# Attention heads ahead of two MLPs, Trainium2: the TensorE's fp32r products and its fp32 products in one stretch each per head, with four score chunks of 384, 384, 384 and 448 columns

## The reference

```
B, H, S, D = 4, 8, 576, 64
scores = where(causal, -1e9, (q @ k.T) / sqrt(D))
a = exp(scores - scores.max(-1));  a /= a.sum(-1) + 1e-9
local = a @ v
phi(x) = where(x > 0, x, exp(x) - 1) + 1
mem_out = (phi(q) @ M_prev) / (phi(q) @ z_prev + 1e-6)
g = sigmoid(beta)
attn = g * mem_out + (1 - g) * local          # [B, S, H * D]
x = (s * relu(attn @ w_in)**2 + b) @ w_out     # first MLP
out = layernorm(solu(x @ v_in)) @ v_out        # second MLP
```

## Time and profile before

| | us |
|---|---|
| median of 3 runs | 821.39 (821.21 to 822.12) |
| profiled execution, its own time | 821.17 |
| profiled execution, span | 819.4 |
| TensorE busy (matmuls) | 810.7 |
| VectorE busy | 510.4 |
| ScalarE busy | 339.6 |
| GpSimd busy | 339.1 |

### The profile page before, as it was taken

One profiled execution on the slowest core, in us unless ns is written; L12 is line 12 of the kernel. 1 busy time (PEld: TensorE's weight loads), 2 busy tenths in 40 slices (PEclk: granted clock), 3 DMA queues, 4 the chain that ended last, 5 costly groups with the idle time before them and its releaser, 6 DMA issues.

```text
span 819.4 us, 14574 instructions
## 1 busy us (share of the span) xinstructions
PE 810.7 (99%) x5630; PEld 704.2 (86%) x5630; DVE 510.4 (62%) x1052; ACT 339.6 (41%) x608; POOL 339.1 (41%) x453
## 2 busy tenths in 40 slices
PE   8999999999999999999999999999999999999998
PEld 7788888888888888888888899999998888888886
DVE  7877777776588653333433353346688977777762
ACT  6766776675422232222322232233436434333431
POOL 6667676676899930000000000005268844443300
PEclk9999999999999999999999999999999999999999
DMA  8587777866134320000000000000111000000001
GB/s 152 128 178 154 173 167 155 178 142 144 53 103 116 95 73 1 1 1 0 1 1 0 1 1 1 1 1 1 52 51 52 26 27 26 26 14 27 26 14 51
DMA packets 86371, 49.45 MB, mean 60 GB/s; under 512 B 65056, under 2 KB 73248, under 8 KB 86304
## 3 DMA queue, kind: packets, MB, share of 16 engines
q1 hardware_dynamic: 83760, 47.94, 24.3%
q10 hardware_dynamic: 2544, 0.59, 0.4%
HBM read 27.28 MB, written 4.72 MB: 39 GB/s over the span
## 4 chain that ended last, share of the span: by engine, by line
PE 96%; DVE 1%; issue 0%; ACT 0%; POOL 0%; POOLq 0%
PE ps_h L1297 8%; PE ps_y L1313 8%; PE ps_h L1298 8%; PE ps_h L1299 8%; PE ps_y L1314 8%; PE ps_y L1312 8%; PE ps_v L678 5%; PE ps_s L591 4%; PE ps_r L1766 4%; PE ps_r L1764 4%; PE ps_r L1765 4%; PE ps_hid L1701 4%; PE ps_hid L1699 4%; PE ps_hid L1700 3%; PE ps_x L657 3%; PE ps_x L658 3%
## 5 line engine op out<-in xcount | busy, mean ns | idle before, releaser
L1414 DVE TENSOR_TENSOR xT<-xT 128x512 f32<-128x512 f32 (+1 forms) x80 | 61.2, 765 | 127.7 <-ACT xT L1372 127.7
L1598 POOL TENSOR_TENSOR win<-stage,win 128x512 fp32r<-128x512 f32 x2 | 2.6, 1296 | 282.4 <-ACT win L1833 282.4
L1314 PE MATMUL ps_y<-g_hi,wout 128*128 128x512 f32 (+1 forms) x320 | 117.5, 367 | 0.0
L1313 PE MATMUL ps_y<-g_lo,wout 128*128 128x512 f32 (+1 forms) x320 | 117.5, 367 | 0.0
L1312 PE MATMUL ps_y<-g_hi,wout 128*128 128x512 f32 (+1 forms) x320 | 117.4, 367 | 0.0
L1378 ACT ACTIVATE g_hi<-xT 128x512 fp32r<-128x512 f32 (+1 forms) x80 | 47.3, 591 | 135.0 <-DVE xT L1416 135.0
L1297 PE MATMUL ps_h<-x_hi,win 128*128 128x512 f32 (+1 forms) x280 | 103.0, 368 | 0.0
L1299 PE MATMUL ps_h<-x_hi,win 128*128 128x512 f32 (+1 forms) x280 | 102.8, 367 | 0.0
L1298 PE MATMUL ps_h<-x_lo,win 128*128 128x512 f32 (+1 forms) x280 | 102.8, 367 | 0.0
L1372 ACT ACTIVATE xT<-ps_h 128x512 f32<-128x512 f32 (+1 forms) x80 | 44.3, 554 | 139.0 <-PE ps_h L1299 137.2
L1419 DVE TENSOR_TENSOR g_lo<-xT,g_hi 128x512 fp32r<-128x512 f32 (+1 forms) x80 | 65.1, 813 | 52.6 <-ACT g_hi L1378 52.6
(11 more groups left out here) (220 smaller groups left out, 1814.6 us busy)
## 6 DMA issues: line engine op xcount, KB each, us to landing
stacked<-cut SPq DMA_DIRECT2D x56, 288.0 KB, 4.8
out<-res SPq DMA_DIRECT2D x18, 256.0 KB, 2.0
v_raw<-in_v SPq DMA_DIRECT2D x32, 128.0 KB, 2.7
stage<-in_moe_w_in SPq DMA_DIRECT2D x16, 256.0 KB, 2.8
stage<-in_moe_w_out SPq DMA_DIRECT2D x16, 256.0 KB, 2.7
k_raw<-in_k SPq DMA_DIRECT2D x28, 128.0 KB, 2.6
q_raw<-in_q SPq DMA_DIRECT2D x28, 128.0 KB, 3.6
stage<-in_moe_w_in SPq DMA_DIRECT2D x4, 512.0 KB, 3.5
```

Of the source, the lines that this page charges most:

```text
L1313: pe.matmul(out, wout[:, f, HI, w], g_lo[:, r, 0:n], start=False, stop=False)
L1314: ins = pe.matmul(out, wout[:, f, LO, w], g_hi[:, r, 0:n], start=False, stop=(f == FT - 1))
L1414: dve.tensor_tensor(r, r, r, ALU.mult).then_inc(square_done, 1)
```

## The change

- `CHUNKS`: key tiles 1 and 2 change places, and tile 0 is split at column 192 in place of 288. The chunks are then 384 (320 + 64), 384 (192 + 192), 384 and 448 columns. `p_order`, `DIAG_AFTER` and GpSimd's waits on `tri_done` follow.
- TensorE's `steps`: chunks 0, 1 and 2, then `second_rows`, chunk 3 and `third_rows` stand together, then the transposes of keys or `memory`, then all of `weigh_values` and `weigh_last`. `turn_queries` comes last in an odd iteration, `turn_output` last in an even one.
- `turn_queries` now waits for `scale_memory` of the same iteration, since `memory` comes ahead of it; `memory` waits for one `copy_queries` less.
- ScalarE takes the four exponentials first. VectorE's `scale_local(pr - 1)` moves from the end of an even iteration to the odd one behind it, between `first_rows` and `second_rows`; `cut_keys` moves behind `third_rows`.

```diff
+    SPLIT = 3 * REST
+    CHUNKS = [[(2, 2 * P, S), (4, 4 * P, S)], [(3, 3 * P, S), (0, 0, SPLIT)], [(0, SPLIT, S)], [(1, P, S)]]
...
-    DIAG_AFTER = [[1, 4], [3, 0], [], [2]]
+    DIAG_AFTER = [[2, 4], [3, 0], [], [1]]
...
         def turn_queries(p):
...
             elif p == 3:
                 pe.wait_ge(t_mem_done, 1)
-            elif p > 3:
+            elif p == 4:
                 pe.wait_ge(k_lo_done, p + 1)
-                need(pe, xT_done, p - 4)
+            elif p > 4:
+                pe.wait_ge(t_mem_done, p - 1)
...
         def memory(p):
...
-            pe.wait_ge(qT_copied, min(p + 3, NPAIR))
+            pe.wait_ge(qT_copied, min(p + 3 if p < 3 else p + 2, NPAIR))
...
                 ahead, here, behind = is_head(h + 2), is_head(h), is_head(h - 1)
+                last_even = h == HEADS - 2
...
                 if here:
                     cross(h, 0)
                     cross(h, 1)
+                    cross(h, 2)
+                if ahead:
+                    second_rows(h + 2)
+                if here and not last_even:
+                    cross(h, 3)
+                if ahead:
+                    third_rows(h + 2)
+
                 if even and is_pair(pr + 3):
                     turn_keys(pr + 3)
                 elif even and is_pair(pr - 2):
                     turn_output(pr - 2)
+                if not even and is_pair(pr + 1):
+                    memory(pr + 1)
+                if behind:
+                    weigh_values(h - 1, (0, 1, 2, 3))
+                if behind and even:
+                    weigh_last(pr - 1)
                 if not even and is_pair(pr + 3):
                     turn_queries(pr + 3)
...
                 if even and is_pair(pr + 3) and is_pair(pr - 2):
                     turn_output(pr - 2)
...
                 ahead = is_head(h + 2)
...
-                if even and is_pair(pr + 3):
-                    cut_keys(pr + 3)
+                if not even and is_pair(pr - 1):
+                    scale_local(pr - 1)
                 if ahead:
                     second_rows(h + 2)
                     third_rows(h + 2)
+                if even and is_pair(pr + 3):
+                    cut_keys(pr + 3)
                 if not even and is_pair(pr + 1) and pr + 1 > 0:
                     scale_memory(pr + 1)
-                if even and is_pair(pr - 1):
-                    scale_local(pr - 1)
```

More of the change, by code:

```diff
@@ L128, in attention @@
     NP = sum(wide)
-    CHUNKS = [[(1, P, S), (4, 4 * P, S)], [(3, 3 * P, S), (0, 0, S // 2)], [(0, S // 2, S)], [(2, 2 * P, S)]]
+    SPLIT = 3 * REST
+    CHUNKS = [[(2, 2 * P, S), (4, 4 * P, S)], [(3, 3 * P, S), (0, 0, SPLIT)], [(0, SPLIT, S)], [(1, P, S)]]
     chunk_width = [sum(hi - lo for _, lo, hi in c) for c in CHUNKS]
     chunk_at = [sum(chunk_width[:c]) for c in range(len(CHUNKS))]
-    p_order = [1, 4, 3, 0, 2]
+    p_order = [2, 4, 3, 0, 1]
     p_at = [sum(wide[i] for i in p_order[:p_order.index(j)]) for j in range(NT)]
-    DIAG_AFTER = [[1, 4], [3, 0], [], [2]]
+    DIAG_AFTER = [[2, 4], [3, 0], [], [1]]
     rows_of = [min(P, S - P * t) for t in range(NT)]
@@ L436, in steps @@
                 if is_head(h + 1):
-                    pool.wait_ge(tri_done, h * NT + 2)
+                    pool.wait_ge(tri_done, h * NT + len(DIAG_AFTER[0]))
                     spread_maxima(h + 1)
@@ L464, in gpsimd @@
         mask_weights(0, 0)
-        pool.wait_ge(tri_done, 2)
+        pool.wait_ge(tri_done, len(DIAG_AFTER[0]))
         spread_maxima(1)
@@ L474, in gpsimd @@
         mask_weights(1, 1)
-        pool.wait_ge(tri_done, NT + 4)
+        pool.wait_ge(tri_done, NT + len(DIAG_AFTER[0]) + len(DIAG_AFTER[1]))
         spread_maxima(2)
@@ L482, in gpsimd @@
         mask_weights(2, 1)
-        pool.wait_ge(tri_done, 2 * NT + 4)
+        pool.wait_ge(tri_done, 2 * NT + len(DIAG_AFTER[0]) + len(DIAG_AFTER[1]))
         spread_maxima(3)
@@ L707, in steps @@
                     turn_output(pr - 2)
+                if not even and is_pair(pr + 1):
[4 more added lines that the diff above has]
+                    weigh_last(pr - 1)
                 if not even and is_pair(pr + 3):
                     turn_queries(pr + 3)
[L710 to L723, removed]
                 if even and is_pair(pr + 3) and is_pair(pr - 2):
                     turn_output(pr - 2)
-                if behind and even:
-                    weigh_last(pr - 1)
                 if last_even:
@@ L943, in steps @@
                     exp_weights(h, 1)
+                    exp_weights(h, 2)
                     if aside:
                         aside()
+                    exp_weights(h, 3)
                 if even and is_pair(pr + 3):
@@ L949, in steps @@
                     copy_output(pr - 2)
-                if not even and is_pair(pr + 3):
-                    copy_queries(pr + 3)
                 if is_pair(pr + 2):
@@ L957, in steps @@
                         feature_relu(pr + 2)
-                if here:
-                    exp_weights(h, 2)
-                    exp_weights(h, 3)
+                        feature_exp(pr + 2)
+                if not even and is_pair(pr + 3):
+                    copy_queries(pr + 3)
                 if even and is_pair(pr + 3) and is_pair(pr - 2):
                     copy_output(pr - 2)
-                if not even and is_pair(pr + 2):
-                    feature_exp(pr + 2)
         def let_go():
```

## The result

The changed kernel takes 835.07 us (median of 4 runs, 834.72 to 835.16) against 821.35 us before (4 runs); the ratio is 1.0164, with a 95% interval of 1.0147 to 1.0182. It is 13.7 us slower. The forecast was 832.3 us, in a range of 825.5 to 837.0.

A forecast was written before the change was run, and what follows sets the result against it. TensorE, which waits for no other engine, was taken to bound the kernel. Grouping -10.9, widths +1.1 and three waits +9.0, +5.9 and +5.8 sum to +10.9 us, giving 832.3 us, range 825.5 to 837.

The forecast's parts named there:

- Grouping, 0.39 per border: TensorE: one group of ps_v products between full-array products less in each of 28 heads, 0.39 us each, -10.9 us.
- The rival by which a border costs no weight load: TensorE: weight loads never run ahead over the full array, a border costs only 0.28 us; 835.4 us, chance 0.02.
- Widths, +1.1: TensorE's chunks: one more narrow piece, limited by weight loads 0.11 us apart, costs 0.04 us per head, +1.1 us.
- Wait 1: TensorE's chunk 2 waits for the exponential of chunk 0, same ps_x bank: 0.32 us in 28 heads, +9.0 us.
- A: The start of chunk 0 on TensorE, from which the prediction counts its times in us.
- Wait 2: Odd iterations: turn_queries on TensorE waits for VectorE's scale_memory to read ps_t, 0.54 us in 11, +5.9 us.
- Wait 3: Even iterations: the turned output on TensorE waits for VectorE's cut_keys, 0.53 us in 11, +5.8 us.
- 0.05 to TensorE: Delay from the end of a producer to TensorE's start, taken as 0.05 us in the sums of the waits.
- The rival "faster": TensorE keeps its pace: the grouping shows and the waits don't; -9.8 us, 811.6 us, chance 0.08.
- a further wait: Maxima, masks or stacked<-cut copies come late and hold up the next iteration, 0.5 us per pair; 838 us, chance 0.06.

The follow-up runs named there:

- widths_only: The kernel before with the new chunk widths alone, TensorE's order untouched: 822.87 us, against 821.4 us before.
- queries_early: The changed kernel with the queries turned, and copied on ScalarE, between chunks 1 and 2 of odd iterations: 825.42 us.
- all_early: both_early with cut_keys back between first_rows and second_rows on VectorE: 817.73 us, ratio 0.9954 to the kernel before.
- local_back: The changed kernel with scale_local back at the end of VectorE's even iteration: 836.09 us.
- both_early: The changed kernel with keys (even iterations) and queries (odd iterations) turned between chunks 1 and 2, their ScalarE readers behind the second exponential: 821.41 us.
- values_by_act: all_early with the three loads of v per pair issued by ScalarE in odd iterations in place of SyncE: 820.98 us.

## Why the prediction was right, and where it was off

The sign, the three waits, their places, their releasers and the sum within 2.8 us were right. By its own steps:

- **Grouping, 0.39 per border.** Measured 0.34, in odd iterations (widths_only 6.10 against queries_early 5.76) and in even ones (6.56 against 6.22 in all_early), so -9.5 us for 28 and not -10.9. The 0.39 is a sum of three readings, of which the group's fixed 0.18 comes from two groups of different length; which of the three is 0.05 too high is not shown. The rival by which a border costs no weight load had 0.28, and its 835.4 us lies nearer to the measured time than my 832.3. It does not get there for its reason: full-array loads do go 0.11 to 0.2 us ahead of their matmuls. The rule that loads overlap running matmuls only when row groups differ (the Trainium skill, "TensorE: Matmul & The Clock Gate", Part 3) does not describe these products. The same Part of the Trainium skill also names a second case, a load into the background weight buffer; no run here tells whether this is it. (That all of them use every row, as the prediction has it, is wrong: L658 in an even iteration uses 69 of 128.)
- **Widths, +1.1.** Measured +1.2 in all, but only about 0.7 of it where the forecast had it (**widths_only**). The agreement is partly luck.
- **Wait 1, 0.32 at A + 1.14.** Chunk 2's load stands at 160.49, A + 1.13, 0.32 late. In heads 26 to 29, where no other wait was added, the four iterations went from 22.51 to 22.43 us, -0.02 each: wait 1 eats the border, as the sum has it (-0.03).
- **Wait 2, TensorE at A + 5.48, for 0.54.** VectorE was done at A + 5.35 (158.07 against A = 152.72), and TensorE started at 158.22, A + 5.50. Waits 1 and 2 together cost 0.94 (6.70 against 5.76 in queries_early), forecast 0.86. I had VectorE's list alone as the cause. **local_back** shows that `add_halves`, done at A + 4.44 there and not by A + 4.3, holds VectorE just as long.
- **Wait 3, TensorE at A + 5.52, for 0.53.** The keys were cut at A + 5.47 as forecast, but TensorE started at A + 5.74. Waits 1 and 3 together cost 0.91 (7.13 against 6.22 in all_early), forecast 0.85.

Where do the missing 2.8 us lie? The forecast amounts to 6.60 us for an odd iteration and 7.02 for an even one; they took 6.70 and 7.13. Over eleven pairs that is 2.3 us. Some 1.5 of it are the waits (0.08 and 0.06 more than forecast), some 0.8 the iterations without their waits (5.76 and 6.22 against 5.74 and 6.17), since a border gives back less. The other 0.5 was not followed.

The term of the waits that was mis-sized is "0.05 to TensorE", which I took from VectorE following ScalarE. For TensorE's transposes it is 0.15, and 0.26 where another wait stands behind the deciding one. In odd iterations most of this was hidden, because VectorE was done 0.08 sooner than I had added up.

The rival "faster" needed VectorE to be done by A + 4.94, and it never was. Where it was brought about, in all_early, the gain was 3.6 us and not 9.8. The copies `stacked<-cut` then came late in some iterations and a pair took 12.3 us on average, where an undisturbed one takes 11.98. I had that only as "a further wait" of the changed kernel, where it did not show; presumably because the longer pairs there give the copies time.

## What to carry to other kernels

Work that stands between a producer and its reader on a full engine is cover, and a new order that groups like with like takes it away. Before grouping, write down for every shared buffer when the reader wants it and when the last of its producers is done, on each engine's own list. Look at the smallest of these slacks, not at the busy shares. Here it was 0.17 us for the turned output, under one border of 0.34. Count every chain that ends at the wait: taking the longest one away gains nothing if a second ends equally late (**local_back**). Fill such a gap with work of the kind that costs no border (full-array transposes between fp32r products), and check that the readers' engines take it up at once: a step placed behind another wait throws away the time that was won.

## What the runs showed of the hardware that I had not expected

- A wait that has long been met still costs TensorE time if it stands behind the one that decides. Moving `k_lo_done` behind `xT_done` cut the distance from VectorE's end to the first transpose from 0.26 to 0.15 us, and 1.0 us of the whole. The wait is an instruction of 51 ns, and two of them start 0.11 us apart. The Trainium skill ("Advanced Engine Details and Errata", Network/Comms) puts the reading of a semaphore from a sequencer at 50-100 ns; the 51 ns of one such instruction lie in that range, and the 0.11 from one to the next just above it.
- What costs at a border is the change to products of 64 weight columns with a tile position, not the change of data type. all_early and both_early put fp32 transposes over the full array between fp32r chunks. Their odd iterations change type as often as before, and still they are a whole border shorter (0.34) for the one group of tiled products less. The two properties, 64 columns and the tile position, were not tried apart.
- TensorE's chunk products start only 0.05 behind their releaser, not 0.15 (the load at 160.49 behind an exponential that ends at 160.44). In the trace no semaphore instruction stands between the two; ahead of the turned queries one does, from 158.11 to 158.16, between VectorE's end at 158.07 and the load at 158.19. That this accounts for the difference was not tried by a run.
- Issuing a load takes longer than its bare 0.5 to 0.6 us when copies are in flight: on ScalarE's queue in values_by_act the three loads of v took 3.2 us (71.70 to 74.89), in the kernel before the same three on SyncE mostly 1.8 (162.07 to 163.89). What lengthens them was not tried apart.
